# A fused attention, Fourier and feed-forward kernel: row sums, hits and masks moved in the order of a head, tables loaded in pieces, output rows one step later

## The reference, cut to what matters

```python
# attention: B=2, H=8, S=768, D=64, 16 centroids
q_assign = argmax(q_n . c_n); k_assign = argmax(k_n . c_n)      # cluster of each row, per head
mask = q_assign[:, :, :, None] == k_assign[:, :, None, :]
scores = where(mask, scale * q @ k.T, -1e9)
attn = exp(scores - max(scores)); attn = attn / (sum(attn) + 1e-9)
x = attn @ v                                                     # (B, S, 512)
# Fourier mix, normalised, a feed-forward layer of 2048
u = x + real(fft(fft(x, axis=1), axis=2))
y = u + relu(norm(u) @ w_ch1) @ w_ch2
# second layer: 1024 wide, a convolution of 3 over tokens as a gate
h = relu(y @ w_in); gate = sigmoid(conv3(h))
out = (h * gate) @ w_out
```

## Time and profile before

| | us |
|---|---|
| median of 3 runs | 702.04 |
| lowest, highest | 700.24, 702.35 |
| the profiled execution | 700.6 |
| its span (first to last instruction) | 698.7 |
| PE busy | 681.3 (98%) |
| DVE busy | 330.6 (47%) |
| ACT busy | 272.6 (39%) |
| POOL busy | 230.6 (33%) |

### The profile page before, as it was taken

One profiled execution on the slowest core, in us unless ns is written; L12 is line 12 of the kernel. 1 busy time (PEld: TensorE's weight loads), 2 busy tenths in 40 slices (PEclk: granted clock), 3 DMA queues, 4 the chain that ended last, 5 costly groups with the idle time before them and its releaser, 6 DMA issues.

```text
span 698.7 us, 9616 instructions
## 1 busy us (share of the span) xinstructions
PE 681.3 (98%) x3666; PEld 553.7 (79%) x3666; DVE 330.6 (47%) x598; ACT 272.6 (39%) x522; POOL 230.6 (33%) x248
## 2 busy tenths in 40 slices
PE   8899999999989999999999999999999999999998
PEld 7677676777766779888888888888888899988876
DVE  4776676766746638753113211131111489933410
ACT  4766666666646632111112111121111377743411
POOL 5645669748566051578500000000150070000000
PEclk7999999999999999999999999999999999999999
DMA  5563444434552020233200000010040520000011
GB/s 172 138 143 89 116 130 106 127 80 118 166 134 65 0 69 31 61 104 107 61 1 0 1 1 0 1 60 1 21 161 1 178 63 1 1 31 30 31 46 46
DMA packets 25917, 47.03 MB, mean 67 GB/s; under 512 B 3728, under 2 KB 10768, under 8 KB 25616
## 3 DMA queue, kind: packets, MB, share of 16 engines
q1 hardware_dynamic: 23392, 38.08, 19.5%
q0 software_dynamic: 2336, 7.95, 3.6%
q10 hardware_dynamic: 144, 0.39, 0.2%
HBM read 35.98 MB, written 3.15 MB: 56 GB/s over the span
## 4 chain that ended last, share of the span: by engine, by line
PE 87%; DVE 7%; ACT 2%; DMA 2%; issue 1%; POOL 1%; SPq 0%; DVEq 0%; POOLq 0%
PE ps L1570 19%; PE ps L1536 19%; PE ps L1618 9%; PE ps L1632 9%; PE ps L1339 9%; PE ps L1325 7%; PE ps L1314 5%; PE ps L1315 4%; DVE row_min L905 1%; DMA q<-mask_r 1%; PE ps L1269 1%; ACT prob L686 1%; PE ps L1416 1%; PE ps L1386 1%; DVE pt L913 1%
## 5 line engine op out<-in xcount | busy, mean ns | idle before, releaser
L1147 DVE SCALAR_TENSOR_TENSOR hid_l<-ps,hid_h 128x512 fp32r<-128x512 f32 x48 | 33.2, 691 | 195.9 <-ACT hid_h L799 195.9
L905 DVE TENSOR_REDUCE row_min<-ps 128x1 f32<-128x768 f32 x96 | 91.5, 953 | 71.5 <-PE ps L1315 71.3
L799 ACT ACTIVATE hid_h<-ps 128x512 fp32r<-128x512 f32 x48 | 28.7, 598 | 223.7 <-PE ps L1536 223.7
L686 ACT ACTIVATE prob<-ps,row_min 128x768 f32<-128x768 f32 x96 | 86.5, 901 | 18.8 <-DVE row_min L905 16.8
L1325 PE MATMUL ps<-cst,prob 128*128 128x128 f32 x576 | 83.8, 275 | 2.4 <-DVE pt L913 0.6
L1314 PE MATMUL ps<-k,q 80*128 80x384 f32 x192 | 75.5, 393 | 5.4 <-DMA q<-mask_r 3.2
L1325 PEld LDWEIGHTS ps<-cst,prob 128*128 128x128 f32 x576 | 69.1, 142 | 11.3 <-issue 7.5
L1570 PE MATMUL ps<-w_h,hid_h 128*128 128x512 f32 x192 | 76.2, 397 | 0.0
L1570 PE MATMUL ps<-w_h,hid_l 128*128 128x512 f32 x192 | 75.5, 393 | 0.0
L1570 PE MATMUL ps<-w_l,hid_h 128*128 128x512 f32 x192 | 74.7, 389 | 0.0
L1339 PE MATMUL ps<-pt,v_n 128*64 128x384 f32 x384 | 68.8, 494 | 0.0
(11 more groups left out here) (175 smaller groups left out, 1369.5 us busy)
## 6 DMA issues: line engine op xcount, KB each, us to landing
w_raw<-in_moe_w_ch SPq DMA_DIRECT2D x24, 256.0 KB, 2.5
raw_d<-in_q SPq DMA_DIRECT2D x8, 384.0 KB, 3.6
v_n<-in_v SPq DMA_DIRECT2D x16, 192.0 KB, 2.5
out<-out_s SPq DMA_DIRECT2D x12, 256.0 KB, 2.0
raw_qk<-in_k SPq DMA_DIRECT2D x15, 192.0 KB, 3.3
raw_qk<-in_q SPq DMA_DIRECT2D x15, 192.0 KB, 3.6
q<-q SPq DMA_DIRECT2D x15, 192.0 KB, 3.1
k<-k SPq DMA_DIRECT2D x15, 192.0 KB, 3.3
```

Source lines behind the costliest of these rows:

```text
L686: nc.scalar.activation(prob[t % 2][:, :, :].rearrange("p (h j) c -> p h (j c)", h=2), ps[:, 2 * (t % 2):2 * (t % 2) + 2, 0:HALF], ACT.Exp, ...
L905: nc.vector.tensor_reduce(row_min[:, col:col + 1], ps[:, 2 * (t % 2):2 * (t % 2) + 2, 0:HALF], axis=AX.XY, op=ALU.min).then_inc(min_ready, 1)
```

## The change

Five edits. ROW_LAG is 3 instead of 2. The token table comes in three pieces for each of its two parts (770 KB in each of the turns 12, 13 and 14) instead of two whole parts in turns 12 and 13. The channel table's DMAs stand ahead of `fold_block(0, 3)` and wait for the scores of heads 0 to 14 (90 tiles), whose buffers they overwrite. The mask: `first_hit` and `masks` on DVE stand at the end of the even head, `turn_mask` on PE behind `fold_o` of the odd head, `store_mask` on ACT one step earlier. `denominator` and `invert` on DVE stand together behind `store_right(m, 0)`. No instruction of computation is added or taken away.

```diff
@@ -48,7 +48,7 @@
-ROW_LAG = 2
+ROW_LAG = 3
@@ -602,18 +602,19 @@ POOL
-                if n in (12, 13):
+                if n in (12, 13, 14):
                     if n == 12:
                         pool.wait_ge(dots_ready, UNITS_M)
-                    part = n - 12
-                    nc.gpsimd.dma_start((seq_h, seq_l)[part][:, :, :],
-                                        seq_tab[:, part, :, :]).then_inc(seq_loaded, 16)
+                    r = n - 12
+                    for part, table in enumerate((seq_h, seq_l)):
+                        nc.gpsimd.dma_start(table[:, r, :], seq_tab[:, part, r, :]).then_inc(seq_loaded, 16)
                 if n == 14:
                     nc.gpsimd.dma_start(seq_fix[:, :], fix_tab).then_inc(fix_loaded, 16)
 
-            fold_block(0, 3)
+            pool.wait_ge(score_ready, NT * (NH - 1))
             nc.gpsimd.dma_start(ch_h[:, :, :], chan_tab[:, 0, :, :]).then_inc(ch_loaded, 16)
             nc.gpsimd.dma_start(ch_l[:, :, :], chan_tab[:, 1, 0:2 * KC, :]).then_inc(ch_loaded, 16)
+            fold_block(0, 3)
             fold_block(1, 3)
@@ -722,14 +723,14 @@ ACT, head
                 exponent(n + 1, 1 - s, 0)
                 store_left(n, 5)
-                step(n + 1, 1 - s, 0)
+                exponent(n + 1, 1 - s, 1)
+                store_left(n + 1, 0)
                 if n % 2 == 0 and u < UNITS_M:
                     store_dots(u)
-                step(n + 1, 1 - s, 1)
                 if n % 2 and u < UNITS_M:
                     store_mask(u)
-                exponent(n + 1, 1 - s, 3)
-                store_left(n + 1, 2)
+                step(n + 1, 1 - s, 1)
+                step(n + 1, 1 - s, 2)
                 step(n + 1, 1 - s, 3)
@@ -1009,21 +1010,16 @@ DVE, head
-                if masking:
-                    first_hit(u)
                 step(n, s, 4)
-                denominator(n, s, 0)
                 if n:
                     store_x(n - 1)
                 minimum(m, 1 - s, 1)
-                invert(n, 0)
                 store_right(n, 5)
-                denominator(n, s, 1)
                 minimum(m, 1 - s, 2)
-                invert(n, 1)
                 store_right(m, 0)
-                if masking:
-                    masks(u)
+                for a in range(2):
+                    denominator(n, s, a)
+                    invert(n, a)
                 minimum(m, 1 - s, 3)
@@ -1035,6 +1031,8 @@ DVE, head, at its end
                 if dotting:
                     weigh_hits(u)
+                    first_hit(u)
+                    masks(u)
@@ -1363,6 +1361,8 @@ PE, head
                 if n:
                     fold_o(n - 1)
+                if n % 2 and u < UNITS_M:
+                    turn_mask(u)
                 step(n, s, 5)
@@ -1371,8 +1371,6 @@
                     turn_dots(u)
-                if n % 2 and u < UNITS_M:
-                    turn_mask(u)
                 step(nxt, 1 - s, 2)
@@ -1487,7 +1485,7 @@ PE
-            pe.wait_ge(seq_loaded, 32)
+            pe.wait_ge(seq_loaded, 32 * R)
```

## The result

The changed kernel takes 690.46 us (median of 4 runs, 689.77 to 691.84) where the kernel before takes 701.72 (4 runs): ratio 0.9845, 95% interval 0.9821 to 0.9869. The forecast was 691.5. The span of the profiled execution fell from 698.7 to 688.9, by 9.8 us, which is the sum that the prediction had; that the two sums agree to the tenth is luck, since some terms came out larger and others smaller.

The account below looks back on a forecast made before the run. PE, busy 98%, bounds the kernel. Gains 4.50 + 0.51 + 2.0 + 1.2 + 0.41 + 1.15 = 9.8 us give 690.8 from the profiled 700.6 or 692.2 from the median 702.04; 691.5 taken, range 688.5 to 697.5.

Parts of the forecast that it names:

- The mask rows: Before head 12's V1, PE stalls on late mask rows; storing and issuing them earlier gains 4.50 us (2.5 to 4.7).
- the thirds: Token table in 770 KB pieces over three heads: cost nothing (0 to 4.5 us, a second stall).
- The low clock behind the stall: Behind PE's stand from 201.7 to 204.8, granted clock 0.57 for 3.6 us, counted within the 4.50 us.
- Head 3: Wait in front of scores (5, 0), taken as the same mask lateness: gain 0.51 us (0 to 0.51).
- The mask's place in the rhythm: Mask transposes moved: V1 to V2 loses 0.37, V2 to V1 gains 0.03; net 0.34 x 6 heads, 2.0 us.
- The sums: Sums and inverses leave DVE's chain in V2 to V1: 0.15 in eight heads without a mask, 1.2 us.
- Channel table: Issued at head 14 on POOL, so PE no longer waits for it: gain 0.41 us (0 to 0.7).
- tail: Row lag three removes PE's lost time in narrow 6: gain 1.15 us (0.9 to 1.25).
- A: Rival: stalls go, but another chain holds PE in every head; gain 6.6, 694.0 to 695.4 us; chance 0.20.
- B: Rival: mask rows stay late and PE stops for head 13; gain 5.3, 695.3 to 696.7 us; chance 0.10.
- C: Rival: DVE block behind weigh_hits outlasts its idle time; gain 4.1, 696.5 to 697.9 us; chance 0.10.
- D: Rival: table pieces stall heads 13, 14 and 15 by 4.5 each; slower, 704.3 us; chance 0.03.

Follow-up runs that it names:

- table late: Kernel before with the second token table's DMA (`seq_l`) in turn 14 instead of 13, nothing else: 696.13 against 701.23 us, ratio 0.9924.
- mask alone: Kernel before with only the mask's edits on DVE, PE and ACT, token table whole, sums in the old place: 694.01 against 700.93 us, ratio 0.9891.
- thirds alone: Kernel before with only the token table sent by thirds, mask still late: 699.13 against 700.93 us, ratio 0.9968.
- lag: Kernel before with only `ROW_LAG = 3`: 699.32 against 700.93 us, ratio 0.9976.
- channel table: Kernel before with only the channel table's DMAs ahead of `fold_block(0, 3)`: 700.01 against 701.23 us, ratio 0.9988.
- sums alone: Kernel before with only `denominator` and `invert` behind `store_right(m, 0)`: 699.04 against 700.93 us, ratio 0.9959.
- the changed kernel again: The changed kernel, nothing altered, measured once more for comparison: 691.60 against 701.34 us for the kernel before, ratio 0.987.
- three blocks: Changed kernel with `store_x` behind `store_right(n, 5)` and the values in three blocks instead of two: 692.14 against 701.34 us for the kernel before, ratio 0.988.

## Why the prediction was right, step by step

**The mask rows: 4.50 forecast, 4.63 measured** (11.54 to 6.91, 0.13 of it by the move of the sums). The cause was right, shown from both sides: take the table away (table late: 7.05) or the lateness of the mask (mask alone: 7.05), and the stall is gone. That the thirds cost nothing was right as well, and in the changed kernel they give nothing either; by themselves they took 0.8 to 2.3 us off the stall, whose size varies. The low clock behind the stall was rightly counted: with the thirds alone 2.25 of waiting cost 3.7.

**Head 3: 0.51 forecast, 0.55 in this profile, nothing in most others.** V2 to V1 there is 8.38 in the profile before, but 7.82 or 7.83 in four kernels that keep the mask late and the sums in place (lag, thirds, channel table, table late). The difference lies in SP's queue. In the profile before, issuing the two rows into k takes 2.15, one of them 1.51 by itself; by thirds it takes 1.23:

```profile
82.47 2.15 SPq L418 DMA_DIRECT2D k<-mask_r  x2
```

```profile
83.78 1.23 SPq L418 DMA_DIRECT2D k<-mask_r  x2
```

So SP begins the last row 0.4 us behind the start of V2 (83.59), where by thirds it begins 0.5 ahead of it (84.90). With the sums alone one issue takes 0.99, the last row begins 0.1 ahead of V2, and the stretch is 7.73, 0.03 over its like. This fits late rows, as read in the earlier trace rows; but the profile names no releaser, and no run set this delay by itself, so it is argued and not shown. What the step had wrong is that it took one execution's wait for a fixed one: one of six profiles with the late mask has it. What makes an issue on SP take 1.51 instead of 0.6 is open.

**The mask's place in the rhythm: 2.0 forecast, 1.56 measured.** V1 to V2 gave the 0.37 of the forecast in all six heads. V2 to V1 grew by 0.11 (7.04 to 7.15), not 0.03: the minimum of (m, 1) waits for scores that the transposes push back (scores done at 187.81, minimum from 187.84 in front of head 11), and `store_right(n, 5)`, for which the last turn waits, stands behind it. So DVE's chain and PE's work add up in part, and taking `store_x` out of that chain left 7.16. 0.26 x 6 = 1.56. I had named the range 7.06 to 7.13 and taken its lower part; 7.15 lies above all of it, though the DVE's 0.15 had left the chain too (with the sums in their old place it is 7.20).

**The sums: 1.2 forecast, about 1.0 measured,** 0.12 or 0.13 in each of eight heads, and by the sums alone in thirteen; in front of head 12 the stall hides it.

**Channel table 0.41 forecast, 0.64 measured; tail 1.15 forecast, 1.35 measured** (142.98 to 141.63). I had taken the channel table's wait as the page shows it, 0.41, but an idle time counts from the end of the matmul before, and a matmul is followed before its end. By starts, the one at 261.71 should have been followed 0.18 later and was followed at 262.47, 0.58 too late. The matmul behind a wait is slower too: the next one starts 0.19 behind it instead of 0.12 here, and 0.34 instead of 0.23 behind 666.58. That makes 0.64 for the table and 1.26 for the tail. The rest of the tail is 0.1 ahead of the first `narrow`: with lag two it comes 50.03 behind the first `widen`, with lag three 54.15, of which one more `widen` is 4.22.

Sum of the traces: 4.63 + 0.55 + 1.56 + 0.85 (sums without head 12, counted above) + 0.64 + 1.35 + 0.23 (an earlier first V1, chance) = 9.8. Without head 3 and the earlier start, which depend on the execution, it is 9.0. The stall, on the other hand, was small in the profile before: in three other kernels that have the whole table right ahead of late rows it makes that stretch 11.68, 11.75 and 13.02, not 11.54. That is 0.1 to 1.5 us more to gain, 9.2 to 10.5 in all. The medians fell by 9.7 (the changed kernel again) and by 11.3; what is over 10.5 is within the interval of the ratio (9.2 to 12.6 us), and no trace accounts for it. The forecast of 691.5 was placed by hand between 690.8 and 692.2, so its nearness to 690.46 is no finer proof than the range.

**The rivals.** A (rhythm unchanged), B (rows late still) and C (DVE's block too long) are refuted by the stretches above; D (three stalls instead of one) by the thirds alone, where V2 to V1 in front of heads 13 and 14 keeps 7.04. For A there is this much: V1 to V2 stays at 6.70 against 6.4 of PE's own work. The expectation for three blocks put that down to the exponents; the one attempt at it cost more than it gave.

## What to carry to other kernels

When a small transfer is late, look at what large one went out just before it, on any queue. Here sending the small one some microseconds ahead removed the whole stall, while cutting the large one removed part of it. Moving instructions pays where they hold the engine that bounds the kernel, so compare the starts of a repeated block with and without them, before and after (7.07 and 6.70 here). And a gap in one of several like places of one profile may be missing in the next execution: look at a second profile before it becomes a term of the sum.

## What had not been expected of the hardware

A wait of PE of 2.25 us was followed by some 3.4 us at the lower clock level (thirds alone, 0.50 to 0.56 in 205.0 to 208.5), as one of 3.2 was by some 3 us (kernel before). Small DMAs between buffers of the core, issued 0.3 us behind a large load from another queue, landed about when the load did (kernel before: the load 6.7 us after its issue, the rows into q 6.1).

The 24 small matmuls that PE runs first on loaded data take 2.88 us in some executions and 5.33 in others, though the code is the same. The rows are from the kernel before and from thirds alone; the granted clock reads 1.00 in 6 to 9 us in both.

```profile
6.47 2.88 PE L1256 MATMUL ps<-cen_b,raw_d 128*128 128x32 f32 x24 [0.57 <-DVE cen_b L899]
```

```profile
6.48 5.33 PE L1256 MATMUL ps<-cen_b,raw_d 128*128 128x32 f32 x24 [0.57 <-DVE cen_b L899]
```

The three profiles with 5.3 in this place have the three latest first V1 (34.28 to 35.04). The 29 runs of the kernel before beside the first experiments spread over 5.2 us (698.73 to 703.88), and this difference of 2.5 can be part of it. What sets it was not tried. The stretch from the first widen to the first narrow varies too (50.03 to 50.80 with lag two), by PE's waits for xt_l.
